# Attention with two gated products: queries, keys, values and weights laid out ahead of the launch, w3 folded by half blocks

## The reference

```python
# q, k, v: (4, 8, 576, 64) float32
q_d = q.reshape(B, H, Sd, 4, D).mean(axis=3)          # the same for k_d, v_d; Sd = 144
out_d = softmax(scale * q_d @ k_d.T) @ v_d            # pooled attention, over 144 positions
mask = abs(pos[:, None] - pos[None, :]) < 4
out_local = softmax(where(mask, scale * q @ k.T, -1e9)) @ v   # each position sees 7 neighbours
x = repeat(out_d, 4, axis=2) + out_local              # then (B*S, H*D) = (2304, 512)
h = ((x @ w1) * (x @ w2)) @ w3                        # w1, w2: 512x1024, w3: 1024x1024
x = h @ w_out                                         # w_out: 1024x512
g = x @ w_in; g = g * sigmoid(g)                      # w_in: 512x2048
return g @ w_out2                                     # w_out2: 2048x512
```

## Time and profile before

| | value |
|---|---|
| median of three runs | 840.68 us |
| the profiled execution | 841.73 us, span 839.9 us |
| PE busy | 816.2 us, 97% of the span |
| DVE, ACT, POOL busy | 609.2, 336.5, 284.1 us |
| granted PE clock, mean | 0.994 |
| read from HBM | 63.44 MB, 81 GB/s over the span |
| first product starts | 173.97 us |

### The profile page before, as it was taken

The page is one execution under the profiler, slowest core; times in us unless marked ns, Lnnn a source line. Parts: engine busy times, 40 slices in busy tenths (PEclk is TensorE's granted clock), DMA queues, the critical chain, the costliest instruction groups (busy, mean ns, idle before and its releaser), DMA issues.

```text
span 839.9 us, 14773 instructions
## 1 busy us (share of the span) xinstructions
PE 816.2 (97%) x5584; PEld 733.6 (87%) x5584; DVE 609.2 (73%) x976; ACT 336.5 (40%) x605; POOL 284.1 (34%) x348
## 2 busy tenths in 40 slices
PE   5899999999999999999999999999999999999998
PEld 4778888788999999999999998898898898988987
DVE  3667779887768676677768876777866778866654
ACT  3645565653225422433226333235333245333231
POOL 5876668843322432233221421320411311411100
PEclk9899999999999999999999999999999999999999
DMA  7856676211110111101112311311511311512202
GB/s 184 214 146 163 153 195 169 61 51 51 51 52 26 51 51 51 51 26 51 50 52 76 101 51 51 101 51 50 176 51 55 96 51 50 176 51 62 64 1 75
DMA packets 128731, 68.98 MB, mean 82 GB/s; under 512 B 63392, under 2 KB 117152, under 8 KB 128672
## 3 DMA queue, kind: packets, MB, share of 16 engines
q1 hardware_dynamic: 128672, 68.18, 28.6%
HBM read 63.44 MB, written 4.72 MB: 81 GB/s over the span
## 4 chain that ended last, share of the span: by engine, by line
PE 90%; DVE 5%; issue 2%; POOL 1%; ACT 0%; DMA 0%; SPq 0%; DVEq 0%; POOLq 0%
PE ps L1054 41%; PE ps L1112 24%; PE ps L1083 12%; PE ps L1213 4%; PE ps L1127 2%; PE ps L1192 2%; PE ps L1176 1%; PE ps L1137 1%; PE ps L1148 1%; PE ps L1167 1%; PE ps L1221 1%; PE ps L1159 1%; DVE wa L750 1%; DVE tr L744 1%; DVE tot L847 0%
## 5 line engine op out<-in xcount | busy, mean ns | idle before, releaser
L1054 PE MATMUL ps<-xb,wa 128*128 128x384 f32 x2016 | 405.4, 338 | 2.4 <-DVE a L882 1.4
L1054 PEld LDWEIGHTS ps<-xb,wa 128*128 128x128 f32 x2016 | 355.0, 188 | 24.6 <-DVE mu L882 2.6
L433 POOL TENSOR_TENSOR rw<-rw 128x256 f32<-128x256 f32 x48 | 42.3, 880 | 443.1 <-DMA rw<-in_moe_w_in 208.6
L882 DVE TENSOR_TENSOR mu<-ps,mu 128x384 f32<-128x384 f32 x132 | 73.3, 555 | 121.0 <-PE ps L1054 120.7
L1083 PE MATMUL ps<-g,r 128*128 128x512 f32 (+1 forms) x576 | 125.0, 338 | 1.8 <-issue 1.8
L644 ACT ACTIVATE a<-a 128x384 f32<-128x384 f32 x72 | 37.9, 526 | 188.6 <-DVE a L882 188.6
L1112 PE MATMUL ps<-w2h_even,g 128*128 128x512 f32 x432 | 113.2, 394 | 0.0
L1112 PE MATMUL ps<-w2h_odd,g 128*128 128x512 f32 x432 | 112.5, 393 | 0.0
L750 DVE TENSOR_TENSOR wa<-rw,wa 128x1024 fp32r<-128x1024 f32 x96 | 108.5, 1131 | 2.6 <-ACT wa L507 2.3
L1083 PEld LDWEIGHTS ps<-g,r 128*128 128x128 f32 x576 | 97.7, 188 | 10.4 <-issue 2.4
L1112 PEld LDWEIGHTS ps<-w2h_odd,g 128*128 128x128 f32 x432 | 79.9, 188 | 11.9
(11 more groups left out here) (86 smaller groups left out, 881.7 us busy)
## 6 DMA issues: line engine op xcount, KB each, us to landing
rw<-in_moe_w SPq DMA_DIRECT2D x48, 256.0 KB, 3.2
rw<-in_moe_w_in SPq DMA_DIRECT2D x48, 256.0 KB, 3.1
w2r<-in_moe_w_out SPq DMA_DIRECT2D x48, 256.0 KB, 2.9
qn<-in_q SPq DMA_DIRECT2D x32, 144.0 KB, 3.0
kn<-in_k SPq DMA_DIRECT2D x32, 144.0 KB, 3.2
vw<-in_v SPq DMA_DIRECT2D x32, 144.0 KB, 2.9
out<-osb SPq DMA_DIRECT2D x18, 256.0 KB, 2.4
wn<-in_moe_w SPq DMA_DIRECT2D x16, 256.0 KB, 3.0
```

The costliest lines, as they stand in the source:

```text
L433: nc.gpsimd.tensor_tensor(blocks[:, 4, :], blocks[:, 0, :], blocks[:, 1, :], ALU.add).then_inc(s1_ready, 1)
L882: nc.vector.tensor_tensor(o, half_bank(k, i), term, ALU.add).then_inc(sum_ready, 1)
L1054: e = nc.tensor.matmul(ps[:, (k + i) % 2, 0:TH], wa[:, k % 2, l, A_SLOT[i], a * P:(a + 1) * P], xb[:, i, r, a, :], start=(i in (0, 1, 4) a ...
```

## The change

The arrays are laid out in `kernel()` by numpy before the launch. Queries and keys come as one array by pair with the head dimension on partitions, so a pair is one transfer of 128 x 1152; so are the grouped values, the value windows, and each half block of w3, already turned. A set of weights for the products is one transfer too.

```diff
-        qn = sb("qn", [PT, 2, CH, 2 * D], where=att)
-        kn = sb("kn", [PT, 2, CH, 2 * D], where=att)
+        qk = sb("qk", [P, 3, 2, S], where=att)
-        pT, pS, pP, pO, pW = 0, 2, 4, 6, 7
+        pS, pD, pP, pO, pW = 0, 2, 4, 6, 7
+        FOLD = 3
+        HALVES = 2 * MT
+        AHEAD = 2 * HP + 1
+            def load_qk(s):
+                after(sp, scored, 2 * (s - 2))
+                sp.dma_start(qk_at(s).rearrange("p c s -> p (c s)"), qk_in[s, :, :]).then_inc(qk_here[s % 3], 16)
+            def load_w3(q):
+                after(sp, w3_lo, q - 1)
+                sp.dma_start(wn[:, q % 2, :], w3_in[q, :, :]).then_inc(w3_here[q % 2], 16)
...
+            act.dma_start(qk_at(1).rearrange("p c s -> p (c s)"), qk_in[1, :, :]).then_inc(qk_here[1], 16)
...
-                    copy_act(gate_a[:, 0:1], ident[0:1, 0:1])
-                    copy_act(r2_block(m, 0), ps[:, pS if last else pW, :]).then_inc(w3o_hi, 1)
+                act.wait_ge(w3_mul, 2 * m + 2)
+                copy_act(r2[:, m, 0, :], ps[:, fold_bank(2 * m), :]).then_inc(w3o_hi, 1)
...
+                    copy_act(od[:, w, :], ps[:, pO, 0:SD]).then_inc(od_ready, 1)
...
-                    nc.vector.tensor_tensor(w3t[:, 1, m4, :].rearrange("p m c -> p (m c)"), ps[:, bank, :],
+                nc.vector.tensor_tensor(w3t[:, 1, m4, :].rearrange("p m c -> p (m c)"), wn[:, q % 2, :],
                                             w3t[:, 0, m4, :].rearrange("p m c -> p (m c)").bitcast(F32),
                                             ALU.subtract).then_inc(w3_lo, 1)
...
+                qs = halves_of(s)
+                scores_local()
+                for q in qs:
+                    multiply(q, 0)
+                if s > 0:
+                    turn_local()
+                scores_down()
+                for q in qs:
+                    multiply(q, 1)
+                if s > 0:
+                    turn_down()
+                    weighted_local_waits()
+                    for q in qs:
+                        multiply(q, 2)
+                    weighted_local()
+                    weighted_down()
+                for q in qs:
+                    multiply(q, 3)
```

More of the change, by code:

```diff
@@ L298, in load_windows @@
[L298 to L319, removed]
-            load_q(0, 0, True)
-            load_k(0, 0, True)
@@ L489, in step @@
-                if isinstance(s, int) and AHEAD < s <= AHEAD + 4:
-                    sums((s - AHEAD - 1) // 2, (s - AHEAD - 1) % 2)
-                if isinstance(s, int) and s in (1, 2):
-                    w_out_low(range(MT // 2 * (s - 1), MT // 2 * s))
-            steps(pool, step)
+                pool.wait_ge(inv_l, s + 1)
+                nc.gpsimd.tensor_tensor(pr, pr, inv[:, u, :, None].broadcast_to([P, 10, BW]), ALU.mult
+                                        ).then_inc(norm_l, 1)
@@ L495, in _ @@
+                if AHEAD <= s < AHEAD + 4:
+                    sums((s - AHEAD) // 2, (s - AHEAD) % 2)
+            for s in range(PAIRS):
+                step(s)
             pool.wait_ge(xb_hi, 3)
@@ L865, in step, with take_local @@
                     nc.vector.reciprocal(invd[:, u, :], totd1[:, u, :]).then_inc(inv_d, 1)
[L866 to L874 removed]
+                def take_local(half):
+                    dve.wait_ge(summed, 2 * (s - 1) + 1)
+                    dve.wait_ge(od_ready, s)
+                    p = s - 1
+                    at = (p % HP) * N + (p // HP) * S + half * HALF
+                    n = HALF // POOL
+                    xf = x[:, :, :].rearrange("p k n -> p (k n)")
+                    nc.vector.tensor_tensor(
+                        xf[:, at:at + HALF].rearrange("p (t f) -> p t f", f=POOL),
+                        ps[:, pP + half, 0:HALF].rearrange("p (t f) -> p t f", f=POOL),
+                        od[:, w, half * n:(half + 1) * n, None].broadcast_to([P, n, POOL]), ALU.add
+                    ).then_inc(x_ready, 1)
@@ L876, in half_bank @@
+                if AHEAD <= s < AHEAD + 4:
+                    dve.wait_ge(x_ready, 2 * 2 * HP)
+                    token_sum(0, s - AHEAD)
+            pool_pair(0)
+            for s in range(PAIRS + 1):
+                step(s)
             def half_bank(k, i):
@@ L1218, in turn_w3 @@
-                def turn_w3(flip, bank):
-                    pe.wait_ge(wn_in[flip[1]], 16 * flip[0] + 16)
-                    for a in range(4):
-                        e = nc.tensor.transpose(ps[:, bank, a * P:(a + 1) * P], wn[:, flip[1], a * P:(a + 1) * P],
-                                                ident[:, :])
-                    e.then_inc(w3_turned, 1)
-                if not turn and not score:
-                    for a in range(4):
-                        multiply(a)
+                if s == PAIRS:
+                    for part in range(4):
+                        multiply(HALVES - 3, part)
@@ L1275, in step @@
                     weighted_local()
                     weighted_down()
-                    multiply(3)
-            steps(pe, step)
+                for q in qs:
+                    multiply(q, 3)
+            warm(8)
+            for s in range(PAIRS + 1):
+                step(s)
             for k in range(SETS):
```

660 lines of the change are left out of this document (291 added, 369 removed).

## The result

The changed kernel takes 832.43 us (median of 4 runs, 831.21 to 834.28). The kernel before, run beside it, takes 840.64 (840.3 to 842.79). The ratio is 0.9899, with a 95% interval of 0.9871 to 0.9926: 8.2 us less. A second series of the same two kernels gave 832.50 and 0.9901 (0.9880 to 0.9922). The forecast was 833.5, so the total was right within 1.1 us. Its two large parts were not: the fill came out worse than forecast and the rest better, and in this execution the two errors nearly cancel (5.8 and 7.1 us).

What follows compares the result with a forecast made beforehand. PE bounds the steady steps and latency the fill. Fill to 52.4, steps 82.1, last step 11.7, bank waits 15.2, other waits 5.5 made 166.9 against 173.97; 7.1 plus 1.3 less 1.0 gave 7.4 gained: 833.5 us, range 823 to 840.

Steps and rivals of the forecast that it cites:

- The products unchanged: Everything from the first product to the end: TensorE-bound, to stay at 666 us.
- Block 0 at 6.5: Fill: the score matmuls of head pair 0 start at about 6.5 us, before at 8.61.
- the rival of the late start: Fill: the 576 KB transfer delays block 0 to 12 us, 5.5 of the gain gone, 839 us; chance 0.16.
- Block 1 at 9.2: Fill: pair 1's score matmuls start at 9.2 us, before at 18.25, because pooled scores have banks of their own.
- The table load paid, block 2 at 21.8, block 3 at 27.7: Fill: ACT's 1.28 us table load stands behind the first subtraction; scores of pairs 2 and 3 start at these times.
- Waits of 5.1 and 4.7 in steps 3 and 4: Fill: the fold waits 5.1 and 4.7 us for the split of w_out, about as the old kernel did.
- The clock, 1.0 us (bounds 0 to 2.1): Fill: slow PE clock behind four waits of 3.4 to 5.6 us takes 1.0 us off the gain.
- A step of PE 7.46: Steady attention steps: pure PE work falls from 9.05 by 1.59 to 7.46 us; steps 5 to 15 take 82.1.
- Bank waits 15.2: Even halves of the fold: six waits for DVE to empty bank pW, 1.6 to 3.4 us each, 15.2 together.
- Other waits 5.5, last step 11.7: After block 5: w3's low part, x and the multiplies cost 5.5 us; the last step takes 11.7.
- the first rival: Steady steps: the w3 split and POOL's multiply miss each other, first product at 159.4 not 166.9, 826 us; chance 0.20.
- The slower rival: Fold of each even half: each of six bank waits grows by 2.1 us, 12.6 in all, 846 us; chance 0.12.

Runs made afterwards that it cites:

- experiment above: Local scores of every pair wait again for the exponentials of the pair before, nothing else changed against the changed kernel; 831.88 us, ratio 0.9891 to the kernel before.
- second execution: Second profiled execution of the changed kernel, from its repeat with no edit; that series measured 832.50 us, ratio 0.9901 to the kernel before.
- `od` in front: Changed kernel with ACT copying the pooled output od right behind the pooled exponentials, before the w_out and weight copies; 828.10 us, ratio 0.9821.
- TensorE kept busy: Changed kernel with dead transposes (46, 40, 22) on TensorE in front of the local scores of pairs 1, 3 and 4; 831.31 us, ratio 0.9879.
- table run: Changed kernel with one ACT exponential of a constant at the start, so its table loads before the first subtraction is done; 831.88 us, ratio 0.9871.

## Why the prediction was right, step by step

- **The products unchanged**: right, 666.09 against 665.93.
- **Block 0 at 6.5**: 6.14. The 576 KB transfer landed in 5.4 to 5.6 us; the rival of the late start is refuted.
- **Block 1 at 9.2**: 8.69, but worth nothing (experiment above). I had put the early block into the fill as one of its causes, without asking when DVE would get to it. What does shorten the fill is not isolated by a run. The traces show block 0 earlier by 2.5 us, the 6.1 us of waits for q's transfers down to 2.3, and no turns.
- **The table load paid, block 2 at 21.8, block 3 at 27.7**: the load is at 11.26 as forecast, and PE's turns at 15.99. Blocks 2 and 3 are at 23.37 and 29.01, because PE's work of step 1 took 7.4 us at the low clock and not 5.9.
- **Waits of 5.1 and 4.7 in steps 3 and 4**: 5.0 and 2.9. The first size was right; of the second I took 1.8 too much. I named the w_out split as the cause, ACT's copies included; about half of the wait comes from where those copies stand. "About as the old kernel did" was a wrong reading: its waits in steps 3 and 4 were 1.5, 0.2 and 0.3 us, and these two steps took 22.4 us, where they now take 29.2 and 25.3 in the two executions. That is why the 11.35 us gained by block 3 (29.01 for 40.36) are 4.6 at block 5.
- **The clock, 1.0 us (bounds 0 to 2.1)**: this is the term of the fill that failed. Beside their waits steps 3 and 4 took 10.6 and 10.7 us of work where 7.8 is the measure at full speed: 5.7 us in this execution, 2.1 in the other, which has only one slow step. The bounds came from a single pair of rows, 1.35 and 0.81 for a block, and priced one block behind each wait, where up to a whole step's work runs slow. So block 5 was at 58.16 and 54.56, not 52.4.
- **A step of PE 7.46**: 7.78 in the steps without a wait, 3.5 us more over eleven. On the chain a part of the fold (three matmuls) takes 0.89 to 0.90 us behind scores, and 0.69 to 0.75 behind turns or weighted sums; the four make 3.25, where they were 2.78 before, and the turns of the probabilities take 0.55 for 0.70. Together that is the 0.32. The old order had two parts in one run (1.38 for both the earlier trace rows), and the new one has different joints. That a piece depends on its neighbour is read from these rows; no run isolates it. Subtracting rows of the chain supposes that it doesn't.
- **Bank waits 15.2**: 7.5 (8.9 in the second execution), in six places as forecast. Quiet ones are 0.8 and not 1.6, because POOL's multiply ends before the totals need the port; those beside token sums are 1.7 and 2.5 and not 3.3.
- **Other waits 5.5, last step 11.7**: the last step took 165.61 - 145.61 - 7.78 - 0.83 = 11.4. What is left of the 107.45 us from block 5 on, after 85.6 + 11.4 + 7.5, is 3.0: 1.1 for `x` in step 12, and 1.6 of half speed in step 13.
- **The sum**: fill 5.8 later than laid out (2.2 in the second execution), the rest 107.45 and not 114.5. Two errors of opposite sign left 1.3 us at the first product (3.6 in the second execution). That the total came within 1.1 us is luck. The method found the places of the bank waits; its sizes were right only on the whole. By the prediction's own sign, "the fill isn't some 10 us shorter", the account of the fill was wrong: it is 4.6 and 8.2 shorter. The steady part had the sign that was forecast, even and odd steps that differ.
- **Small slips**: 834.33 less 1.05 is 833.3, not 833.5, and the slope between the two reduces gives 1.30 for the pooling, not 1.35 (it took 1.34).
- **The collisions**: right as a mechanism (L388 1.52 for 1.26), wrong in what hangs on them: not the 7.5 us of the first rival. The slower rival named the right place, and the run with w3's pass moved shows that one DVE pass of 0.66 us in the wrong place is enough to take back the gain (ratio 0.9991), though not for the 846 us of that rival.

## What to carry to other kernels

When an engine's work is taken away, the next bound is what it used to cover: list for each wait what stood between release and need, and look whether an independent piece can be put there (here five turns in front of the fold, 4.8 us, and no work added). Look for bulk copies that stand in front of a small one which others wait for; moving the small one was worth 4.3 us by the medians. And an early start of one engine is a gain only from the moment at which the engine behind it gets there.

## What the runs showed of the hardware

A DVE pass over 72x4 elements (TENSOR_SCALAR, both ends in SBUF) took 0.15 us where no POOL instruction had just started, and 1.20 (changed kernel) and 1.19 us (`od` in front, L709 at 48.19) where one had started 0.08 and 0.09 before it; each time it ended within 0.03 of POOL's. The first of them, DVE and POOL:

```profile
14.76 1.20 DVE L736 TENSOR_SCALAR totd<-totd 72x4 f32<-72x4 f32 x1 [0.16 <-ACT prob_d L455]
...
14.68 1.26 POOL L388 TENSOR_TENSOR prob<-prob,inv 128x640 f32<-128x640 f32 x1 [3.50 <-DVE inv L732]
```

The Trainium skill, "SBUF — State Buffer", section "Who interferes with whom", says that whoever issues first holds the shared port pair for the whole instruction; by that rule the trace agrees where POOL is first. Where DVE is first it shows less than the rule: L388 at 90.02 lost 0.26 us (1.52 for 1.26), while L688 still ran for 0.41.

PE's speed after a wait is not the same in each execution: after 2.88 and 2.91 us of waiting, with the same work behind it, it was low once and high once, and so it was after 2.25 (TensorE kept busy) and 2.26 (second execution). Nor does the record of it always fit the durations. For 15 to 20 us the one execution shows 0.50 (the 1.2 GHz level) and the other 1.00 (2.4 GHz), but in both the five turns at 15.97 and 15.99 take 1.33 us, against 0.71 at full speed. Windows of PE in the one and in the other:

```profile
15.00:20.00 5.00, 4.01 (x31) 0.50 0.41 149
```

```profile
15.00:20.00 5.00, 4.03 (x33) 1.00 0.42 148
```

So I read the speed from the durations of a known group. The mean over an execution fits the times of the changed kernel (0.992 to 0.994 goes with 830.33 to 831.52 us, 0.981 to 0.988 with 833.47 to 835.13), but not those of the table run, where 0.983 and 0.984 go with 831.62 and 830.61.
